# First expert layer of a fused attention and mixture-of-experts kernel: three steps are placed elsewhere in their queues, and two row tiles get other buffers

## The reference

```
def _moe_ref(x, w_gate, w_noise, noise, w1, w2):        # E = 8 experts, 2 for each token
    logits = x @ w_gate
    noisy_logits = logits + np.log1p(np.exp(x @ w_noise)) * noise
    top2 = np.argpartition(-noisy_logits, 2, axis=1)[:, :2]
    top2_w = softmax of the two chosen noisy logits
    for e in range(E):
        for k in range(2):
            mask = top2[:, k] == e
            h = np.maximum(x[mask] @ w1[e], 0.0)         # 512 -> 1024
            out[mask] += top2_w[mask, k, None] * (h @ w2[e])   # 1024 -> 512
```

## Time and profile before

| | us |
|---|---|
| median of 3 runs | 679.68 (679.19 to 680.46) |
| the profiled execution, device time | 680.44 |
| its span | 678.7 |
| PE busy | 640.8 (94% of the span) |
| PEld busy | 581.7 (86%) |
| DVE busy | 328.6 (48%) |
| ACT busy | 275.7 (41%) |
| POOL busy | 188.1 (28%) |
| chain that ended last, share of PE | 80% |
| the same, DVE / DMA / issue | 7% / 4% / 3% |

### The profile page before, as it was taken

One profiled execution on the slowest core, in us unless ns is written; L12 is line 12 of the kernel. 1 busy time (PEld: TensorE's weight loads), 2 busy tenths in 40 slices (PEclk: granted clock), 3 DMA queues, 4 the chain that ended last, 5 costly groups with the idle time before them and its releaser, 6 DMA issues.

```text
span 678.7 us, 11243 instructions
## 1 busy us (share of the span) xinstructions
PE 640.8 (94%) x3866; PEld 581.7 (86%) x3867; DVE 328.6 (48%) x681; ACT 275.7 (41%) x529; POOL 188.1 (28%) x199
## 2 busy tenths in 40 slices
PE   7989999899999999999999999998989999999981
PEld 6989999898999999999999998987767888788861
DVE  4466646586465527264452724566767222442220
ACT  5678866443344234243433523234516122522110
POOL 2500100127361633516153331101643122121010
PEclk9999999999999999999999999998989999999996
DMA  7878721354594546646364611515559311001000
GB/s 213 273 256 250 262 85 58 103 210 130 178 235 149 101 140 155 188 144 171 103 134 149 155 20 20 153 62 177 150 168 340 113 44 50 20 31 48 15 32 11
DMA packets 51089, 89.84 MB, mean 132 GB/s; under 512 B 7919, under 2 KB 14063, under 8 KB 51040
## 3 DMA queue, kind: packets, MB, share of 16 engines
q1 hardware_dynamic: 41872, 69.21, 30.8%
q0 software_dynamic: 9168, 19.97, 13.5%
HBM read 73.13 MB, written 17.02 MB: 133 GB/s over the span
## 4 chain that ended last, share of the span: by engine, by line
PE 80%; DVE 7%; DMA 4%; issue 3%; ACT 2%; SPq 1%; POOL 0%; ACTq 0%; DVEq 0%; POOLq 0%
PE banks L1058 6%; PE banks L1057 6%; PE banks L1076 6%; PE banks L996 5%; PE banks L997 5%; PE banks L999 5%; PE banks L801 5%; PE banks L829 4%; PE banks L1344 4%; PE banks L1339 4%; PE banks L1340 4%; PE banks L1367 3%; PE banks L1371 3%; PE banks L1368 3%; PE banks L813 2%
## 5 line engine op out<-in xcount | busy, mean ns | idle before, releaser
L1821 DVE TENSOR_TENSOR split<-stage,split 128x2048 fp32r<-128x2048 f32 x32 | 73.3, 2290 | 42.2 <-ACT split L1451 42.1
L996 PE MATMUL banks<-xTs,split 128*128 128x416 f32 (+1 forms) x256 | 88.7, 351 | 1.6 <-issue 1.6
L997 PE MATMUL banks<-xTs,split 128*128 128x416 f32 (+1 forms) x256 | 86.4, 342 | 0.0
L648 POOL DMA_INDIRECT x_moe<-rows,dst_idx x25 | 50.3, 2013 | 114.9 <-DVE rows L2271 112.9
L1057 PE MATMUL banks<-hTs,split 128*128 128x416 f32 x224 | 79.9, 357 | 0.0
L1058 PE MATMUL banks<-hTs,split 128*128 128x416 f32 x224 | 78.6, 351 | 0.0
L1586 ACT ACTIVATE hTs<-banks 128x416 fp32r<-128x416 f32 x56 | 29.0, 518 | 85.4 <-PE banks L999 85.4
L1451 ACT ACTIVATE split<-stage 128x2048 fp32r<-128x2048 f32 x32 | 60.9, 1908 | 0.5 <-DMA stage<-w1a 0.5
L1709 ACT ACTIVATE hTs<-banks 128x512 fp32r<-128x512 f32 x28 | 16.5, 598 | 105.1 <-PE banks L1354 105.1
L999 PE MATMUL banks<-xTs,split 128*128 128x416 f32 (+1 forms) x256 | 56.2, 341 | 0.0
L801 PE MATMUL banks<-k_sb,q_sb 128*128 128x260 f32 (+2 forms) x192 | 49.5, 384 | 3.4 <-DMA k_sb<-k_w 2.0
(11 more groups left out here) (371 smaller groups left out, 1313.6 us busy)
## 6 DMA issues: line engine op xcount, KB each, us to landing
stage<-w1a SPq DMA_DIRECT2D x16, 1024.0 KB, 7.3
stage<-w2a SPq DMA_DIRECT2D x16, 1024.0 KB, 5.5
k_sb<-k_w SPq DMA_DIRECT2D x12, 520.0 KB, 4.9
raw<-w1b SPq DMA_DIRECT2D x4, 1024.0 KB, 6.1
raw<-w2b SPq DMA_DIRECT2D x4, 1024.0 KB, 8.8
q_sb<-q_t SPq DMA_DIRECT2D x24, 128.0 KB, 4.1
x_attention<-rows SPq DMA_DIRECT2D x12, 256.0 KB, 6.0
split<-x_moe SPq DMA_DIRECT2D x12, 256.0 KB, 3.7
```

The source lines that it names most:

```text
L648: pool.indirect_dma_start(out=x_dram[1], out_offset=rows_at(dst_idx[0], early_dst, e, k), in_=y_lines(e, k), in_offset=None, compute_op=AL ...
L996: pe.matmul(psum, piece(slot, 0, o + c * FH), xTs[:, 0, c, 0:cols], start=(c == 0), stop=False)
L997: pe.matmul(psum, piece(slot, 1, o + c * FH), xTs[:, 0, c, 0:cols], start=False, stop=False)
L1821: dve.tensor_tensor(split_chunk(e % 2, 1, c), staged_chunk(e % 2, c), split_chunk(e % 2, 0, c).bitcast(F32), ALU.subtract).then_inc(low_do ...
```

## The change

Four things are moved, all in the first expert layer.

1. On PE, `x1_transposes(1, 3)` stands before `rest_first(1)` and not behind it; on ACT, `x1_high_part(1, 3)` stands before `rest_relu_part(1)`.
2. On PE, the register load of the overflow count stands before expert 1's first piece, behind a wait on `fresh_ready[0]`; the branch stays where it was.
3. The last two row tiles of expert 6 are scaled into `x_rows[:, 2]` and `x_rows[:, 3]`, and `y_scale` for them waits until expert 7's x rows are turned, where it waited for a scatter. `y_room` is moved to where DVE can call it too.
4. On DVE, `second_router` stands ahead of `first_layer_low(2, 2)` and `first_layer_low(2, 3)`, behind the four `x1_low_part(2, k)`.

```
+        def y_room(n):
+            if n >= nth_sub(E - 1, 0):
+                return last_rows[:, n - nth_sub(E - 1, 0)]
+            return x_rows[:, n - nth_sub(E - 2, 0)] if n >= nth_sub(E - 2, 2) else y_rows[:, n % 2]
...
-            def y_room(n):
-                return y_rows[:, n % 2] if n < nth_sub(E - 1, 0) else last_rows[:, n - nth_sub(E - 1, 0)]
...
             def over_layer():
-                over = pe.value_load(used[0:1, 0, 0:1], min_val=0, max_val=OVER_TILES)
                 with pe.If(over > 0):
...
             x1_transposes(1, 2)
+            x1_transposes(1, 3)
             rest_first(1)
-            x1_transposes(1, 3)
+            pe.wait_ge(fresh_ready[0], 1)
+            over = pe.value_load(used[0:1, 0, 0:1], min_val=0, max_val=OVER_TILES)
             for e in range(1, E):
...
                 x1_high_part(1, 2)
+                x1_high_part(1, 3)
                 rest_relu_part(1)
-                x1_high_part(1, 3)
...
-                if n >= 2:
+                if e == E - 2 and k >= 2:
+                    dve.wait_ge(tx1, nth_sub(E - 1, SUBS))
+                elif n >= 2 and e < E - 1:
                     dve.wait_ge(scattered1[n % 2], 16 * (n // 2))
-                dve.tensor_scalar(y_rows[:, n % 2], rows_in,
+                dve.tensor_scalar(y_room(n), rows_in,
...
                         for k in range(SUBS):
                             x1_low_part(e + 1, k)
+                        if e == 1:
+                            second_router()
                         for c in (2, 3):
                             first_layer_low(e + 1, c)
-                    if e == 1:
-                        second_router()
```

## The result

| | before | after |
|---|---|---|
| median of 7 runs each, us | 679.68 (678.48 to 681.92) | 675.55 (675.15 to 678.56) |
| ratio after / before, 95% interval | | 0.9932 [0.9913, 0.9952] |
| profiled execution, device time | 680.44 | 675.41 |
| its span | 678.7 | 673.6 |

The kernel is 4.1 us faster in the median, where 3.4 was forecast: 675.55 against 676.3, inside the range of 674.8 to 678.2. The profiled executions differ by 5.0 us. As will be seen, 3.7 of these are the four edits, and some 1.6 go with the clock in the second layer, which no run ties to the edits.

A forecast was written before the change was run, and what follows sets the result against it. PE was taken as the bound, so changes pay only where it stalls. The terms 0.9 + 0 + 0 + 1.24 + 1.23 = 3.4 us, counted from the 679.68 median, gave 676.3 us, range 674.8 to 678.2.

The forecast's parts named there:

- Edit 1: Before expert 1's first piece: PE's stall for DVE's low part of sub-tile 3 goes, worth 0.9 us (0.79 to 1.03).
- Edit 2a: Before expert 1's first piece: the register load hides in the sequencer's wait, costing 0 us (bounds 0 to 0.8).
- Edit 2b: At expert 7's start: up to 0.8 us won, lost again before its second `back`; 0 at the end.
- The worry that the branch holds PE until its queue is empty: At expert 7's start: the stall at 413 us would then stay, with the same sum.
- Edit 3: Before expert 7's fourth `back`: y_scale(6, 2) no longer waits for a scatter, worth 1.24 us (1.06 to 1.30).
- The margin: At expert 7's fourth `back`: scaling done at 423.45 us, wanted at 424.05, so 0.6 us left over.
- Edit 4: Before back(1, 1), expert 1's second: router constants no longer delay y_scale(1, 0), worth 1.23 us.
- rival (b): At expert 7's start: Edit 2b counts after all, 0.8 us more, giving 675.5 us; chance 0.07.
- rival (c): Behind the first layer: PE's lower clock gives the gains back, 678.4 to 679.8 us; chance 0.08.
- the time from the fourth `back` to the end: From expert 7's fourth `back` to the kernel's end: same time as before; growth would count against the prediction.
- no drop at 504: Near 504 us: PE's clock doesn't drop, 1.7 us less, giving 674.6 us; chance 0.04.
- a next wait in place of a gain: At one of the three gains: the next wait replaces it, sum 2.2 to 2.5 us, 677.2 to 677.5; chance 0.17.

The follow-up runs named there:

- undo_load: Changed kernel with PE's register load back ahead of the branch behind expert 6: 676.9 us, ratio 0.9935.
- later_low_old_load: Changed kernel with DVE's low part of expert 7's last chunk behind expert 6's four y_scale and the register load back ahead of the branch: 678.97 us, one execution.
- undo_turn: Changed kernel with the turn of expert 1's sub-tile 3 behind rest_first(1) again, on ACT too: 678.11 us, ratio 0.996.
- six_loads: Changed kernel with the register load made six times at its new place: 683.74 us, one execution.
- short_body: Changed kernel with the loop in PE's never-entered overflow branch left out: 676.34 us, one execution.
- undo_buffers: Changed kernel with expert 6's last two tiles scaled into y_rows again, waiting for a scatter: 677.26 us, ratio 0.9944.
- undo_constants: Changed kernel with second_router() behind both low parts again: 678.28 us, ratio 0.9965.
- load_alone: Kernel before with only the register load moved ahead of expert 1's first piece: 689.41 us, one execution on a slow occasion.
- changed_again: Changed kernel unaltered, run again on a slow occasion: 684.71 us, ratio 0.9949.
- changed_third: Changed kernel unaltered, run once more as a measure: 676.01 us, ratio 0.9914.
- later_low_part: Changed kernel with DVE's low part of expert 7's last chunk moved behind expert 6's four y_scale: 684.08 us, ratio 0.9934.

## Why the prediction was right

**Edit 1, the turn.** Forecast 0.9 (0.79 to 1.03) with the stall gone; measured 0.94 at expert 1, 1.03 at expert 2. Undoing it alone costs 0.93 at expert 1 and 1.14 by the end of the layer, 0.11 over the upper bound. The sequencer's wait was to end by 164.5 and ended at 164.7, because DVE's low part came at 163.79; with 1.4 us to spare that had no effect.

**Edit 2a, the load's new place.** Forecast 0 (0 to 0.8); it is 0. The two kernels with and without it agree to 0.01 us at expert 1, and six loads cost 0.92 where one costs nothing.

**Edit 2b, the load gone from the branch.** Forecast 0 with a gain of up to 0.8 at 413 that comes back as a stall of 0.5 to 0.8 before the second `back`. Measured 0.86 won from expert 6's start to expert 7's, a stall of 0.69, and -0.06 in all. The rival that it counts after all (0.8 more) is excluded by undo_load, and the reason against it by the kernels with the low part moved. The worry that the branch holds PE until its queue is empty didn't come true: PE ran without a stall at expert 7's start while the branch took 3377 ns. The stall there isn't gone for good, though. Ten profiles have the long branch without the load ahead of it: in two there was no stall (branches of 3377 and 3398 ns), in the other eight one of 0.19 to 0.51 us (3552 to 3878 ns). The stall is what the branch takes beyond some 3.37 us.

**Edit 3, the buffers.** Forecast 1.24 (1.06 to 1.30); 1.23 between the second and the fourth `back`. By undoing it is 0.96, with a scatter 0.36 us quicker. The margin was worked out as 0.6 us; PE had no stall.

**Edit 4, the constants.** Forecast 1.23; 1.24 at the `back`, and 1.34 by expert 3's start. That 0.11, 0.13 of the turn (1.03 at expert 2 against 0.9) and 0.09 behind the fourth `back` are the difference between the 3.4 of the sum and the 3.7 measured by the end of the layer; part of it is that the first turns behind a stall are 0.06 longer, which the sum counted only for edit 3. The constants had "almost 1" us to spare, and the row gives 0.96.

**The number.** The four edits give 3.7 us, so 679.68 - 3.7 = 676.0 us, inside the forecast's own 675.7 to 676.9. The measured 675.55 is outside of that and nearest to the 675.5 of rival (b), which the traces exclude: here the median alone would have pointed to the wrong cause. That all stays in the range owes something to its width. The prediction's sum for rival (c) is also off: one stretch of 1.7 us more is 676.3 + 1.7 = 678.0, two are 679.7, where it has 678.4 to 679.8; the first would have been inside the range.

**A sign that failed.** The prediction wanted the time from the fourth `back` to the end unchanged. To the end of PE's last matmul it was 239.34 us before and 237.48 after, 1.86 less. What follows is the larger part of it.

**What was given a small chance and happened.** The prediction gave 0.04 to "no drop at 504", worth 1.7 us. In the profiled execution of the kernel after that is what happened. It is no effect of the four edits in the sense of a path: from the second layer's first products of hTs to the end of PE's last matmul it took 171.58 us before and 170.02 after, with no edit in between. The clock from 495 to 515, in later_low_old_load and in the kernel after:

```profile
495.00:515.00 20.00, 17.24 (x84) 13.93 (x85) 13.13 (x29) 5.89 (x6) 4.16 (x5) 0.91 0.79 280
```

```profile
495.00:515.00 20.00, 17.14 (x92) 13.79 (x91) 12.36 (x27) 9.19 (x10) 3.85 (x6) 1.00 0.88 319
```

Four profiled kernels have the drop (before, undo_turn, six_loads, later_low_old_load), and the distance is 171.57 to 171.62 us in them. Ten don't; it is 169.89 to 170.06 in nine, and 170.56 in short_body. So the drop goes with some 1.6 us, near the 1.7 that was worked out from the earlier trace rows. The six profiles of kernels with every edit in place and one load are without it, but with six loads it is there, and undo_load, undo_buffers, undo_constants and load_alone are without it too. The time at which the second router starts doesn't order them either: undo_turn, 277.71 us from the start, has it, and undo_buffers, 277.53, has not.

What orders them is where the lower clock lies. Every trace has an earlier stretch at 1.2 GHz near the end of the first layer; in the kernel before it begins at 470.47 us and has ended by 477.3:

```profile
470.50:477.20 6.70, 6.14 (x73) 5.71 (x73) 6.13 (x16) 3.45 (x5) 3.11 (x1) 0.50 0.63 211
```

Counted from the second router's first turns, which lie ahead of it, this stretch begins after 30.75 us in undo_turn, 31.10 in six_loads, 31.11 in the kernel before and 31.46 in later_low_old_load: the four with the drop. In short_body it is 31.52, and in the other nine 31.79 to 32.92 (32.57 in the kernel after). The drop near 504, where there is one, begins 34.1 us after the earlier stretch began, in all four. So the two falls keep their distance from each other and not from the program, and where they lie against it separates the profiles with the drop from those without. That is an order found in fourteen traces, with only 0.06 us between 31.46 and 31.52, and not an experiment. The three executions of the changed kernel have 32.18, 32.57 and 32.92; whether the change makes the drop rarer is open all the same, since the kernel before has one profile and undo_turn, one edit away, has the drop. That it was absent here is luck as far as the prediction goes.

In time, the median fell by 4.1 here, 3.4 in changed_again and 5.1 in changed_third. The distances give 3.7 by the end of the first layer; what is left, from 1.4 more to 0.3 less (in changed_again the distance itself was only 2.95), is of the size by which the medians of the kernel before differ (679.68 beside the first runs of the changed kernel, 681.08 beside changed_third), so its cause stays open.

The remaining rivals, a next wait in place of a gain and gains given back by the clock, did not come true in the profiled execution. No stretch of PE in the first layer behind an edit got longer, except at expert 7 as forecast.

## What to carry to other kernels

Price a stall by the distance between starts where it is and where the same pair runs freely, and ask of each repaired stall which wait on the next `back` (or its like) is already due: three of four stalls here were worth about their full size and the fourth nothing, and the trace of before had the row that said so. A sequencer that is ahead of its engine hides register loads and the start of a branch; put them where its next wait is long anyway. An edit that a second bound makes worthless gets its worth when that bound goes, so the two belong in one trial. And before a difference of 1 or 2 us is given to an edit, compare the stretches at the lower clock in both traces: one of them was worth as much as half of this change.

## What the runs showed of the hardware that I had not expected

**The length of a branch over a long body.** On PE's sequencer the same untaken body costs 3352 to 3878 ns over thirteen profiles (three executions of the changed kernel: 3377, 3702 and 3777), and 231 ns when the body is cut short. The rows give a time to jump over code, not its cause; that new instructions have to be fetched would fit and was not tested apart. The Trainium skill (Advanced Engine Details and Errata, Control Flow Timing) gives about 108 ns for a compare-and-branch; short_body comes within a factor of about two of it, and every other kernel here is thirty times above it or more.

**A register load is cheaper when repeated.** 488 to 495 ns for the first, 301 to 302 for those right behind it, with 0.7 us from one to the next, its register steps included.

**Starts that shift without any change in the code.** The first matmul of `rest_first(0)` started between 159.07 and 161.76 us in ten of the executions, and between 160.89 and 166.08 in load_alone, six_loads, later_low_part and changed_again, where PE stood still for 1.4 to 6.7 us before it with "issue" or DVE's part as releaser. All of that lies ahead of the change, and is why the comparison counts from there. The long ones also cost behind themselves: in six_loads, after 2.19 us of idle time, the granted clock was 0.57 from 163 to 167 us and the wide matmuls stood 0.43 us apart, where they stand 0.23 apart at 1.00.

**The same program at different clocks.** The kernel before, in 28 runs, had a mean granted clock of 0.979 in five of them, at 682.6 us in the mean, and 0.985 in eleven, at 680.8; single runs don't follow it, though: three of the eleven took 682.9 to 683.3. The Trainium skill (TensorE: Matmul & The Clock Gate, What's actually happening) has the clock follow how busy PE has been; that the drop near 504 is there in one execution and not in another, with the same stall ahead of it, agrees with that only if something besides the program decides when it falls. The traces above show as much: the falls keep a distance of their own, and their place against the program differs by up to 2.2 us from one profile to another. What sets that place no run here shows. changed_again was to show whether its executions fall into levels by granted clock; they do so loosely, from 678.0 us at 0.987 to 688.1 and 688.6 at 0.975, with 681.2 to 685.9 between.
